# Block-causal attention with two feed-forward layers: one wait for each matmul on TensorE, and late items' keys rounded ahead of their queries

## The reference

```python
# attention: batch 4, 8 heads, 576 positions, head width 64
scores = scale * np.matmul(q, k.transpose(0, 1, 3, 2))
mask = block_i >= block_j                     # blocks of 64 positions
scores = np.where(mask, scores, -1000000000.0)
scores = scores - np.max(scores, axis=-1, keepdims=True)
attn = np.exp(scores)
attn = attn / (np.sum(attn, axis=-1, keepdims=True) + 1e-09)
x = np.matmul(attn, v)                        # then as (2304 tokens, 512)
# first layer: w_in (512, 2048), w_out (2048, 512)
h = x @ w_in
g = np.where(h >= 1, h, np.where(h <= -1, 0.0, (h + 1) ** 2 / 4))
x = g @ w_out
# second layer, weights of the same shapes
h = x @ w_in
out = (h * np.cos(h)) @ w_out
```

## Time and profile before

| | |
|---|---|
| median of 3 runs | 1045.59 us (1045.02 to 1050.85) |
| the profiled execution | 1051.79 us |
| its span, first to last instruction | 1049.6 us |
| PE busy | 1001.9 us, 95% |
| DVE / ACT / POOL busy | 657.0 / 590.8 / 426.5 us |
| mean granted clock of PE | 0.981 of full speed |
| attention alone | to about 60 us |
| attention beside the first layer | to about 540 us |
| second layer | from about 650 us |

### The profile page before, as it was taken

How to read it: one execution, slowest core, us unless ns; L and a number is a source line. 1 busy time by engine, 2 the same in 40 slices (tenths; PEclk the granted TensorE clock), 3 DMA queues, 4 the chain that set the end, 5 groups by cost and what they waited for, 6 DMA issues and landing times.

```text
span 1049.6 us, 19879 instructions
## 1 busy us (share of the span) xinstructions
PE 1001.9 (95%) x7360; PEld 943.1 (90%) x7360; DVE 657.0 (63%) x1422; ACT 590.8 (56%) x1232; POOL 426.5 (41%) x446
## 2 busy tenths in 40 slices
PE   4688999999999999999999999999999999999997
PEld 3578999999999999999999998999999999999995
DVE  5567777766766767666732378656565555656553
ACT  5567776766666666666633356544444444445442
POOL 3559765555555554655522221222222222222211
PEclk9579999999999999999999999999999999999999
DMA  4335321221211212121200144010110101001000
GB/s 133 104 118 157 98 90 65 72 70 49 92 49 53 89 49 72 70 72 65 69 31 22 41 161 162 1 40 0 40 40 0 40 0 40 21 19 40 0 21 21
DMA packets 30886, 62.28 MB, mean 59 GB/s; under 512 B 3680, under 2 KB 11872, under 8 KB 30816
## 3 DMA queue, kind: packets, MB, share of 16 engines
q1 hardware_dynamic: 29664, 57.16, 17.1%
q10 hardware_dynamic: 1152, 4.19, 1.1%
HBM read 51.90 MB, written 9.44 MB: 58 GB/s over the span
## 4 chain that ended last, share of the span: by engine, by line
PE 79%; DVE 9%; ACT 5%; issue 3%; POOL 1%; DMA 1%; ACTq 0%; POOLq 0%; DVEq 0%
PE hidden L1090 33%; PE acc L1107 18%; PE acc L1115 12%; PE heads_out L1036 4%; PE scores L1001 4%; PE turned L1019 3%; PE scores L1002 3%; DVE neg_max L800 1%; PE heads_out L1019 1%; DVE x_lo L879 1%; PE hidden L1073 1%; DVE wout_lo L865 1%; DVE work L885 1%; ACT probs L616 1%; DVE pt_lo L817 1%
## 5 line engine op out<-in xcount | busy, mean ns | idle before, releaser
L543 POOL TENSOR_TENSOR g_lo<-work,g_hi 128x512 fp32r<-128x512 f32 x144 | 187.9, 1305 | 450.7 <-ACT g_hi L713 450.7
L1090 PE MATMUL hidden<-x_hi,win_hi 128*128 128x256 f32 x1136 | 323.5, 285 | 2.8 <-DVE work L912 1.2
L1090 PE MATMUL hidden<-x_hi,win_lo 128*128 128x256 f32 x1136 | 317.9, 280 | 0.0
L1090 PE MATMUL hidden<-x_lo,win_hi 128*128 128x256 f32 x1136 | 317.9, 280 | 0.0
L1090 PEld LDWEIGHTS hidden<-x_hi,win_hi 128*128 128x128 f32 x1136 | 214.3, 189 | 7.6 <-issue 2.0
L1090 PEld LDWEIGHTS hidden<-x_lo,win_hi 128*128 128x128 f32 x1136 | 214.2, 189 | 3.3
L1090 PEld LDWEIGHTS hidden<-x_hi,win_lo 128*128 128x128 f32 x1136 | 216.4, 190 | 0.0
L1115 PE MATMUL acc<-g_hi,wout_hi 128*128 128x256 f32 x576 | 167.4, 291 | 0.3 <-ACT y_stage L696 0.3
L1115 PE MATMUL acc<-g_lo,wout_hi 128*128 128x256 f32 x576 | 160.6, 279 | 0.0
L1115 PE MATMUL acc<-g_hi,wout_lo 128*128 128x256 f32 x576 | 160.5, 279 | 0.0
L513 POOL TENSOR_SCALAR probs<-probs,row_inv 64x576 f32<-64x576 f32 (+2 forms) x160 | 107.4, 675 | 121.6 <-DVE row_inv L812 120.8
(11 more groups left out here) (91 smaller groups left out, 1830.1 us busy)
## 6 DMA issues: line engine op xcount, KB each, us to landing
qk_raw<-qk_late SPq DMA_DIRECT2D x32, 448.0 KB, 3.2
qk_raw<-qk_early SPq DMA_DIRECT2D x32, 256.0 KB, 2.6
v_raw<-v_late SPq DMA_DIRECT2D x32, 160.0 KB, 3.3
x_raw<-x_scratch SPq DMA_DIRECT2D x9, 512.0 KB, 3.5
out<-y_stage SPq DMA_DIRECT2D x36, 128.0 KB, 2.4
x_raw<-w_in SPq DMA_DIRECT2D x8, 512.0 KB, 3.6
y_stage<-w_out SPq DMA_DIRECT2D x8, 512.0 KB, 3.5
x_scratch<-y_stage ACTq DMA_DIRECT2D x8, 512.0 KB, 2.7
```

Source lines behind the costliest of these rows:

```text
L543: nc.gpsimd.tensor_tensor(g_lo[:, m % G_RING, :], work[:, m % 2, :], g_hi[:, m % G_RING, :], ALU.subtract).then_inc(g_lo_made, 1)
L1090: last = nc.tensor.matmul(into, w[:, p, c, half * P:(half + 1) * P], x[:, c, :], start=(i == 0), stop=(i == len(products) - 1))
```

## The change

The matrix multiplications and their order on PE stay as they are. Three things change.

One: a wait is left out where another wait implies it, and of those that stay, all but a few sit alone on a matmul. Some are for that taken at an earlier matmul: `steps_ahead` takes `v_lo_made` ahead of `weigh` (early items beside the layer), `heads_read` ahead of a late item's second turn, and `pt_lo_made` ahead of its third, each at the last matmul before the half unit's steps; `hidden_ahead` and `use_ahead` take `hidden_read`, and `g_lo_made` or `wout_lo_made` at a tile's first pair, at the last but one matmul of the unit before. In the program as built, 154 of PE's rows of matmuls had one wait and 390 more than one; now it is 648 and 20.

Two: `score` waits for `k_lo_made` at the first matmul that reads `k_lo`, and no more at the one that reads `k_hi`.

Three: in `AT`, `k_hi` of late items goes from slot -10 to -11, the slot of `q_hi`.

```diff
-    "turn_c": (0, 0, 19), "weigh": (18, 18, 21), "k_hi": (-9, -9, -10), "q_hi": (-9, -8, -11),
+    "turn_c": (0, 0, 19), "weigh": (18, 18, 21), "k_hi": (-9, -9, -11), "q_hi": (-9, -8, -11),
...
+def banks_seen(n):
+
+    before = n - 2 if n < ALONE else n - 1
+    last = "inv_c" if late(before) else "inv_b"
+    return n < 2 or slot_of(last, before) - sum(slots_of(m) for m in range(before, n)) <= slot_of("q_lo", n)
...
             def score(n, i):
                 e = i - tiles_of(n)[0]
-                pe.wait_ge(q_lo_made, n + 1)
-                pe.wait_ge(k_lo_made, n + 1)
-
-                if late(n):
-                    pe.wait_ge(exp_made, first_tile(n) + (2 if i == 4 else 0))
-                elif n > ALONE:
-                    pe.wait_ge(exp_made, first_tile(n - 1) + e + 1)
-                elif n > 1:
-                    pe.wait_ge(exp_made, first_tile(n - 1 if n < ALONE else n))
+
+
+                if e == 0:
+                    pe.wait_ge(q_lo_made, n + 1)
+                    if not banks_seen(n):
+                        pe.wait_ge(exp_made, first_tile(n))
+                elif e == 2:
+                    pe.wait_ge(exp_made, first_tile(n) + 2)
...
                     nc.tensor.matmul(into, q_tile, k_hi_of(n)[:, first:end], start=True, stop=False)
+                    if e == 0:
+                        pe.wait_ge(k_lo_made, n + 1)
...
                 pe.wait_ge(probs_made, first_tile(n) + e + len(tiles))
-
-                if e == 1:
-                    pe.wait_ge(heads_read, n)
-                elif e == 2:
-                    pe.wait_ge(pt_lo_made, first_turn(n) + 1)
-                elif user_before(n) >= 0:
-                    pe.wait_ge(pt_lo_made, first_turn(user_before(n) + 1))
...
+            def steps_ahead(n, k):
+
+                for m, j in near(n, k):
+                    if kind(m) == 1 and j == slot_of("weigh", m):
+                        pe.wait_ge(v_lo_made, m + 1)
+                    if late(m) and j == slot_of("turn_b", m):
+                        pe.wait_ge(heads_read, m)
+                    if late(m) and j == slot_of("turn_c", m):
+                        pe.wait_ge(pt_lo_made, first_turn(m) + 1)
...
                 pe.wait_ge(pt_lo_made, first_turn(n) + (3 if late(n) else 1))
-                pe.wait_ge(v_lo_made, n + 1)
-                if user_before(n) >= 0:
-                    pe.wait_ge(heads_read, user_before(n) + 1)
+                if kind(n) == 0:
+                    pe.wait_ge(v_lo_made, n + 1)
...
+            def hidden_ahead(t, m):
+
+
+                pe.wait_ge(hidden_read, PAIRS * t + m + 1)
+
+            def use_ahead(t, p, first):
+
+                if p == 0:
+                    pe.wait_ge(g_lo_made, PAIRS * t + p + 1 + 2)
+                elif first:
+                    pe.wait_ge(wout_lo_made, p + 1)
...
-                if half == 0:
-                    pe.wait_ge(hidden_read, PAIRS * t + m + 1)
...
+                    if i == len(products) // 2 - 1:
+                        ahead_of_half(beside, 2 * u)
                     if i == len(products) // 2:
                         beside_half(beside, 2 * u)
+                    if i == len(products) - 2 and ahead is not None:
+                        ahead()
+                    if i == len(products) - 1:
+                        ahead_of_half(beside, 2 * u + 1)
...
                     for a in range(TOK // P):
                         for i, (w, g) in enumerate(parts):
+                            if a == 1 and i == 1 and ahead is not None:
+                                ahead()
```

More of the change, by code:

```diff
@@ L1008, in turn @@
                 pe.wait_ge(probs_made, first_tile(n) + e + len(tiles))
-                if e == 1:
-                    pe.wait_ge(heads_read, n)
-                elif e == 2:
-                    pe.wait_ge(pt_lo_made, first_turn(n) + 1)
-                elif user_before(n) >= 0:
-                    pe.wait_ge(pt_lo_made, first_turn(user_before(n) + 1))
                 at = 0
-                for i, j in ([(0, 0), (1, 0), (1, 1)] if not late(n) else [(tiles[0], j) for j in range(tiles[0] + 1)]):
+                chunks = [(0, 0), (1, 0), (1, 1)] if not late(n) else [(tiles[0], j) for j in range(tiles[0] + 1)]
+                for i, j in chunks:
                     q = rows_of(i)
@@ L1063, in beside_half, with ahead_of_half @@
                         attention(n, k)
+            def ahead_of_half(beside, half):
+                if beside:
+                    for n, k in beside[half]:
+                        steps_ahead(n, k)
             def begin_hidden(c):
@@ L1093, in make_hidden, with use_hidden @@
                     last.then_inc(hidden_made, 1)
-            def use_hidden(t, p, half, second, beside=None, u=0):
-                if half == 0:
+            def use_hidden(t, p, half, second, beside=None, u=0, ahead=None):
+                if half == 0 and p == 0:
+                    pe.wait_ge(acc_read, t + 1)
+                elif half == 0:
                     pe.wait_ge(g_lo_made, PAIRS * t + p + 1 + 2)
-                    if p == 0:
-                        pe.wait_ge(acc_read, t + 1)
                 slot = p % G_RING
@@ L1113, in use_hidden @@
                         for i, (w, g) in enumerate(parts):
+                            if d == KC // 2 - 1 and i == 2:
+                                ahead_of_half(beside, 2 * u)
+                            if d == KC - 1 and i == 1 and ahead is not None:
+                                ahead()
+                            if d == KC - 1 and i == 2:
+                                ahead_of_half(beside, 2 * u + 1)
                             into = acc[:, d // 2, (d % 2) * TOK:(d % 2 + 1) * TOK]
@@ L1126, in tile @@
                     m = s + LAG
[L1127 to L1135 removed]
+                    if second and u == 4 * (PAIRS - LAG - 1):
+                        pe.wait_ge(half_lo_made[1][1], PAIRS - 1)
+                    if second and u == 4 * (PAIRS - LAG) + 1:
+                        pe.wait_ge(half_lo_made[1][1], PAIRS)
                     if u in (made_at(s, heads) - 1, made_at(s, heads)):
@@ L1138, in tile @@
                             if to_second and m >= PAIRS and half == 0:
-                                for h in range(2):
-                                    pe.wait_ge(half_lo_made[0][h], m - PAIRS + 1)
-                            if heads and t == 0 and m < PAIRS and half == 0:
+                                pe.wait_ge(half_lo_made[0][1], m - PAIRS + 1)
+                            if first and m < PAIRS and half == 0:
                                 pe.wait_ge(win_lo_made, m + 1)
-                            make_hidden(t, m, half, beside, u)
+                            make_hidden(t, m, half, beside, u, ahead_of(u + 1))
                     else:
-                        if heads and t == 0 and half == 0:
-                            pe.wait_ge(wout_lo_made, s + 1)
-                        use_hidden(t, s, half, second, beside, u)
+                        if first and s == 0 and half == 0:
+                            pe.wait_ge(wout_lo_made, 1)
+                        use_hidden(t, s, half, second, beside, u, ahead_of(u + 1))
                     beside_half(beside, 2 * u + 1)
@@ L1155, in _ @@
                     attention(n, k)
+            hidden_ahead(0, LAG)
             for t in range(BESIDE_TILES):
```

22 lines of the change are left out of this document (12 added, 10 removed).

## The result

The changed kernel takes 1112.8 us (1110.73 to 1113.31, 4 runs) where the kernel before takes 1045.3 (1044.64 to 1050.85) on the same chip: a ratio of 1.063, with a 95% interval from 1.0591 to 1.0668. It is 6% slower. I had predicted 1046.5 us, and had given a chance of 0.05 to anything slower by over 1%.

The account below looks back on a forecast made before the run. It took TensorE as the bound, busy for 95% of the span. Terms -1.7 - 1.5 + 1.0 + 0.5 + 2.3 + 0.3 = +0.9 us on 1045.6 gave 1046.5 us, range 1041.5 to 1052.

Parts of the forecast that it names:

- keys rounded ahead of queries on ACT: Late items: `q_hi` and `q_lo` 0.58 us later, PE waiting longer for `pt_lo`; 2.3 us on, bounds nil to 18.
- (b): Rival at late items: DVE, waiting for `q_hi`, blocks `pt_lo` behind it; 1056.7 us at most, or 1064; chance 0.2.
- Single waits at the third score tile: Third score tile on PE: late exponential no longer costs a second wait; 1.7 us off, bounds nil to 2.5.
- `k_lo_made` at its matmul: Late items' score: the `k_hi` matmul runs while POOL still makes `k_lo`; 1.5 us off, bounds 0 to 2.2.
- `pt_lo_made` one matmul ahead: Last turn of late items: wait held one matmul earlier, turn 0.12 us later; 1.0 us on, bounds nil to 2.5.
- `hidden_read` ahead at the second layer's first pair: Near 655 us: the wait sits ahead of two more matmuls of 512 columns; 0.46 us on.
- The copy of `acc`: ACT at 347 us: the copy moves 0.58 us back and PE, which needs it, loses 0.3 us.
- (a): Rival: the gains hold and the shift of ACT and DVE finds gaps, without costs; 1041.7 us; chance 0.22.
- (c): Rival on PE's queue: each removed wait cost 0.09 us even with data there, some 370; -33 us, 1012; chance 0.02.
- (d): Rival: late waits are simply late at another matmul, difference under 0.5 us either way; 1045.6 us; chance 0.06.

Follow-up runs that it names:

- the seventh experiment: The changed kernel with late items' `q_lo` on DVE a scaled copy of the raw queries, one input in place of two: 1096.77 us, ratio 1.0484.
- the fastest version: The changed kernel with late items' `k_hi` back at slot -10 and the `pt_lo` wait back at the third turn: 1042.64 us, ratio 0.998.
- Keys back: The changed kernel with `k_hi` of late items back at slot -10, all its waits kept: 1044.53 us, ratio 0.9993.
- the third experiment: The changed kernel with POOL starting a late item's `k_lo` only when its `q_lo` is done: 1051.62 us, ratio 1.0057.
- the eighth experiment: The changed kernel, swap included, with the wait for `pt_lo` back at the third turn of late items: 1094.25 us, ratio 1.0457.
- the fifth experiment: The changed kernel with POOL's `k_lo` of late items a scaled copy with one input, without the subtraction: 1064.3 us, ratio 1.0171.

## Why the prediction was wrong

**The failed step is the price of the swap, "keys rounded ahead of queries on ACT": +2.3 us, bounds 0 to 18.** The sign of this term and its chain were right: `q_lo` later by about half a microsecond, `pt_lo` behind it in DVE's queue, PE waiting for that `pt_lo`. What failed is one silent assumption: that `q_lo` keeps its 0.49 us wherever it lies. I moved it by 0.58 us and did not look at what POOL does there. It measured 2.14 us on average, and PE waited for `pt_lo` in all 31 items, 42.5 us in total, not for 0.58 us more in a few of seven. By the runs the swap alone costs 50 to 54 us, and with the early wait 68. Rival (b) is half of it: DVE's queue did stop at `q_lo`. But (b) had DVE wait for `q_hi`, which it did for 0.60 us an item, and not be held by POOL once `q_lo` had begun; its largest price, 31 x 0.58, had the same fixed length in it, and its sign, longer waits at the third score tile, isn't in PE's list. That PE's clock falls in a stretch with such stops was in no term at all; it is 24 of the 70 us.

**What the trace of before could have told.** An early item's `q_lo` lies beside its `k_lo` and takes 0.83 us, where it takes 0.42 when no POOL row is under way. It ends 0.29 us after POOL's `k_lo` (DVE, then POOL):

```profile
129.83 0.83 DVE L789 SCALAR_TENSOR_TENSOR q_parts<-qk_raw,q_parts 64x256 fp32r<-64x256 f32 x1
```

```profile
129.64 0.73 POOL L506 TENSOR_TENSOR k_lo<-qk_raw,k_hi 128x256 fp32r<-128x256 f32 x1
130.36 1.00 POOL L513 TENSOR_SCALAR probs<-probs,row_inv 128x128 f32<-128x128 f32 x2
```

And at the place itself, item 53 before, the row that `q_lo` was to slide past stood 0.07 us after it, with a length that was already too long (1.04 us; 0.74 after):

```profile
413.22 1.04 POOL L513 TENSOR_SCALAR probs<-probs,row_inv 64x576 f32<-64x576 f32 x1 [2.27 <-DVE row_inv L812]
414.22 1.41 POOL L506 TENSOR_TENSOR k_lo<-qk_raw,k_hi 128x576 fp32r<-128x576 f32 x1
```

A lead of 0.07 us decided which of the two engines is held. If `q_lo`, moved to 413.73, is kept out until `k_lo` is over, it ends near 414.22 + 1.41 + 0.29 = 415.92, 2.28 us later than it did (413.64). Less the 0.45 us for which DVE stood idle in most items, 1.8 us reach `pt_lo` and the turn, in 31 items: 57 us. This estimate could have been made blind, but only as an upper bound, because the rows of before don't show a `q_lo` that is held through two POOL rows. They show the reverse. In the pair above POOL's `probs` stands directly behind `k_lo` (130.36), and `q_lo` was let in ahead of it. So it was in seven late items, in which `q_lo` began beside `v_lo` or `g_lo`; here it ends 0.34 us after POOL's first row, and `probs` is the one that takes longer (DVE, then POOL):

```profile
206.02 0.65 DVE L789 SCALAR_TENSOR_TENSOR q_parts<-qk_raw,q_parts 64x320 fp32r<-64x320 f32 x1
```

```profile
205.45 0.88 POOL L519 TENSOR_TENSOR v_parts<-v_raw,v_parts 128x320 fp32r<-128x320 f32 x1
206.31 0.99 POOL L513 TENSOR_SCALAR probs<-probs,row_inv 64x576 f32<-64x576 f32 x1
```

With `q_lo` let in between `probs` and `k_lo`, it would have ended near 413.22 + 0.74 + 0.35 = 414.31, 0.67 us later; less 0.45, and for 31 items, that is 7 us. Read without the result, the trace gives 7 to 57 us for the term that was put at 2.3.

The Trainium skill states the mechanism (SBUF — State Buffer, SBUF: two separate sides): DVE and GpSimd share a pair of ports under an exclusive lock; a DVE instruction with two inputs in SBUF (against a GpSimd one that reads SBUF), or in a two-port mode, and a GpSimd instruction don't overlap, and whichever starts first keeps the pair to its end. The rows agree in kind: `q_lo` ahead, `probs` takes 1.02 us in place of 0.74; `probs` ahead, `q_lo` takes 2.14 in place of 0.49. The scaled copy of the seventh experiment has one input and was held as well; that it takes 0.32 us where the row with two inputs takes 0.49 for the same 64x320 fits a two-port mode but doesn't show it. DVE rows that read PSUM are not held: before, all 32 `pt_lo` of a late item's first turn (384 columns) begin beside a POOL row and take 0.55 us; after, 29 of them begin with POOL idle and take 0.55 too.

**Single waits at the third score tile, -1.7, and `k_lo_made` at its matmul, -1.5: right in kind.** In the fastest version item 47's exponential ends at 353.89 (353.70 + 0.19) and its third tile starts 0.06 us later, in place of 0.14:

```profile
353.70 0.19 ACT L623 ACTIVATION_READ_ACCUMULATOR probs<-scores,neg_max 128x1 f32 x1
```

```profile
353.95 0.40 PE L1007 MATMUL scores<-k_hi,q_parts 128*128 128x288 f32 x1
```

Item 43, as in the earlier trace rows: `k_lo` ends at 306.02 and its own matmul starts 0.05 us later, with the other 0.24 us ahead of `k_lo`'s end.

```profile
304.61 1.41 POOL L513 TENSOR_TENSOR k_lo<-qk_raw,k_hi 128x576 fp32r<-128x576 f32 x1
```

```profile
305.78 0.45 PE L1007 MATMUL scores<-k_hi,q_parts 128*128 128x384 f32 x1
306.07 0.44 PE L1010 MATMUL scores<-k_lo,q_parts 128*128 128x384 f32 x1
```

Together -3.2 was expected; between matmuls 960 and 3840 this version gains 1.9 us in its one trace, so the terms were too large, and how the 1.9 divide between the two isn't measured. (The prediction calls 0.30 us the most that a `k_lo` stall gives and then reckons with 0.33, which makes 0.1 us.)

**`pt_lo_made` one matmul ahead, +1.0 (0 to 2.5): right while `pt_lo` is on time, wrong with the swap.** Keys back, the runs with and without it differ by 1.9 us between 960 and 3840, and by 1.9 in their medians; these come from two chips, and their ratios to the kernel before (0.9993 and 0.998) have intervals that overlap. With `pt_lo` two microseconds late it is 15 to 18.

**`hidden_read` ahead at the second layer's first pair, +0.5: right.** Between matmuls 4870 and 4890 the fastest version loses 0.45 us, the changed kernel 0.40; 0.46 was worked out. The kernel with the swap alone, without this wait, loses 0.00. It isn't without exception: the third experiment has the wait and gains 0.28 there.

**The copy of `acc`, +0.3: right.** In the changed kernel this copy (347.29 before) ends at 373.53 (372.52 + 1.01), PE's matmul on `acc` starts 0.05 us later, and the distance to the kernel before grows there by 0.24 us, from 24.69 to 24.93. **Rivals:** (a), gains without costs at 1041.7, isn't the change, but comes nearest to the fastest version (1042.64). (c) is refuted by the version with keys back: it has the change's waits, and is within 0.3% of the kernel before, not 33 us faster. (d) put the late waits at another matmul for under 0.5 us, and the eighth experiment measured 15 to 18 for that.

## What to carry to other kernels

When an edit moves an instruction in time, its duration moves too: look at what the neighbouring engine runs at the new place, and find in the trace a pair of the same two kinds that already overlaps. For DVE and POOL on SBUF tiles, a lead of 0.07 us decided which engine is held, and the one that is held can be kept out through several rows of the other. So a POOL sequence without gaps is a bad neighbour of a DVE instruction that stands ahead of PE's next operand. And count a stall of PE at more than its length: in three traces with the swap (alone, with `pt_lo` waited for at the turn, and as changed) each microsecond of standing came with 0.3 to 0.6 us of lower clock (382 x 0.03 = 11, 15 and 24 us for 43, 43 and 42). No run says why, and the share differs from kernel to kernel.

## What the runs showed of the hardware

- A held DVE instruction isn't always let in between two POOL instructions that follow each other. In the changed kernel `q_lo` began while POOL was in `probs` in 29 late items and was held through `k_lo` as well in all of them, in four through `g_lo` too (3.19 to 3.22 us). These followers have two inputs and begin 0.21 to 0.66 us after `q_lo`. With `probs`, of one input, as the follower, `q_lo` was let in ahead of it in all seven late items of the kernel before (0.13 to 0.43 us after `q_lo`). The `k_lo` of one input in the fifth experiment let it in 11 times (0.47 to 0.66 us) and kept it out 18 times (0.21 or 0.22 us). What decides, the kind of the follower or the moment, no run separates; one early item of before lets `q_lo` in ahead of a `k_lo` of two inputs (97.28 us).
- One input on either side was enough to collide.
- In the second layer the one trace of the kernel before has 324 matmuls in 50 us, and the traces of all other kernels 328 to 332 (850 to 900 us), at a granted clock of 1.00 in both. Among them is the kernel with the swap alone, whose code for the second layer is that of before. The traced execution of before took 6.2 us more than its median, which fits. So the 7 us are no effect of the waits; what makes the pace differ isn't known.
- A wait whose data are in time costs nothing that these runs can tell: 154 and 390 matmuls with one and with several waits became 648 and 20, and with the keys back the ratio is 0.9993 (0.997 to 1.0017).
